# The start row of the routing counts as a 128-row bf16 multiply instead of a one-row fp32 one

## The chip, the cores and the metric

The kernel runs on one core of one Trainium2 chip. The metric is the device time in microseconds (us); a lower time is better. The kernel before took 638.41 us, the median of three runs (637.21 to 638.51).

## The reference

Three stages follow one another: an attention with a sliding window and four sink keys (2 x 8 heads, 768 positions, head size 64), a mixture of 8 experts with a capacity, and a dense two-layer block with a leaky activation. The change touches the second stage, where each of 1536 tokens goes to one expert, greedily by the size of its logit, and no expert takes more than 192:

```python
cap = N // E
logits = x @ w_gate
order = np.argsort(-logits.flatten())
for idx in order:
    tok, e = (int(idx) // E, int(idx) % E)
    if assigned[tok] >= 0 or counts[e] >= cap:
        continue
    assigned[tok] = e
    counts[e] += 1
for e in range(E):
    mask = assigned == e
    h = np.maximum(x[mask] @ w1[e], 0.0)
    out[mask] = h @ w2[e]
```

The third stage is `(g @ w_out)` with `h = x @ w_in` and `g = max(h, 0) + alpha * min(h, 0)`.

## The kernel before

The program is written engine by engine, and the order of each engine's instructions is the order in the code; semaphores join the engines. Nothing is moved by a planner.

The greedy loop is done in eight rounds, r = 0 to 7. After each round one more expert is full. A round needs, for each free token, how many free tokens with a larger logit want each expert. VectorE compares the tokens' keys, one block of 128 tokens (a column c of 12) after another, into the 0/1 matrix `beats` (with `ties` for equal keys), and TensorE multiplies these with `want`, a 0/1 matrix of 128 x 9 for each block, and adds the results up in one PSUM region, `COUNTS` (12 blocks of 9 numbers, 108 columns). `count(r, c)` holds the 13 small matmuls of a column (L1392, L1394). Round 0 does the same by pieces, in `count_first_round` (L1397).

Before the first column, one matmul opens the accumulation with a start row: each of the 128 output rows gets the same 108 numbers, for each expert the number taken so far plus 1 - 192, and -3072 in the ninth place of each block. It is L1400 in round 0 and L1389 in rounds 1 to 6 (round 7 counts nothing), so it runs seven times. Its weights are `ones_row`, one row of 128 fp32 ones, and its moving data is `start_row`, one row of 108 fp32 numbers. GpSimd writes both once, among the constants in `routing_consts` (L498 to L519), during the attention. VectorE rewrites the expert part of `start_row` at the end of each round in `fill_expert` (L1048), from the loads in PSUM. TensorE, VectorE and ScalarE wait for all 23 constants (`consts_ready`) after the attention.

Where the rounds lie: rounds 0 and 1 come after the attention, with little else for TensorE to do; matmuls on zeros (`keep_clock`, L1233) are put between. From there on the rounds are woven into the matmuls of the experts and of the dense block, which go in four groups j of two experts. Round 2 begins after the fourth product of expert 1 (`routing_beside_expert`, L1522), round 4 after the fourth product of expert 3, and round 6 after the fourth of expert 5; rounds 3 and 5 begin in the dense block of group 0 and of group 1, at step f = 8 (`routing_beside_ffn`, L1562). L1505 is the first matrix of an expert, L1514 its second, L1602 the dense block's up projection, L1617 its down projection. `ones`, a 128 x 128 tile of bf16 ones, is there already: it is the weight of the sums over tokens in `before_and_loads` (L1445).

Of the kernel before, what the change touches and what calls it, by code (L numbers as in the profile page):

```python
# [19 lines left out]
BF16 = mybir.dt.bfloat16  # L20
# [7 lines left out]
N, DM = B * S, H * D  # L28
E, FE, FF = 8, 1024, 2048
P = 128  # L30
CAP = N // E
QB = S // P
STEPS = B * QB
NT = N // P
# [24 lines left out]
def program(nc, q_t, k_t, k_sink, v_rows, v_sink_d, wg_d, w1_d, w2_d, w_in_d, w_out_d, alpha_d, out, n_sink, window):  # L59
# [9 lines left out]
    with ctx:  # L69
# [10 lines left out]
        tri_before = sb("tri_before", [P, P], BF16)  # L80
        tri_after = sb("tri_after", [P, P], BF16)
        ones = sb("ones", [P, P], BF16)
        ones_row = sb("ones_row", [1, P])
        logit = sb("logit", [P, NT, E])
        zeros = sb("zeros", [P, 512], BF16)
        alpha = sb("alpha", [P, FC])
# [2 lines left out]
        full = sb("full", [P, E])  # L89
        full_pen = sb("full_pen", [P, E])  # L90

        start_row = sb("start_row", [1, NT, E + 1])
        free = sb("free", [P, NT])
        cap_val = sb("cap_val", [P, NT])
        expert_no = sb("expert_no", [P, NT, E])
# [368 lines left out]
        def _(pool):  # L464
# [33 lines left out]
            def routing_consts():  # L498

                nc.gpsimd.memset(tri_before[:, :], 1.0).then_inc(consts_ready, 1)  # L500
                nc.gpsimd.memset(tri_after[:, :], -1.0).then_inc(consts_ready, 1)
                affine(tri_before[:, :], ALU.is_gt, 0.0, [[1, P]], 0, -1, consts_ready, 4 + 2 + 1)
                affine(tri_after[:, :], ALU.is_gt, 0.0, [[-1, P]], 0, 1, consts_ready, 5 + 2 + 1)
                nc.gpsimd.memset(ones[:, :], 1.0).then_inc(consts_ready, 1)
                nc.gpsimd.memset(ones_row[:, :], 1.0).then_inc(consts_ready, 1)
                nc.gpsimd.memset(one[:, :], 1.0).then_inc(consts_ready, 1)
                nc.gpsimd.tensor_copy(ident_half[:, :], ident[:, :]).then_inc(consts_ready, 1)
                nc.gpsimd.iota(slot_iota[:, :], [[1, CAP]], base=1, channel_multiplier=0,
                               allow_small_or_imprecise_dtypes=True).then_inc(consts_ready, 1)
                nc.gpsimd.iota(expert_no[:, :, :], [[0, NT], [-1, E]], base=E, channel_multiplier=0,  # L510
                               allow_small_or_imprecise_dtypes=True).then_inc(consts_ready, 1)
                nc.gpsimd.memset(full[:, :], 0.0).then_inc(consts_ready, 1)
                nc.gpsimd.memset(full_pen[:, :], 0.0).then_inc(consts_ready, 1)
                nc.gpsimd.memset(start_row[:, :, 0:E], 1.0 - CAP).then_inc(consts_ready, 1)
                nc.gpsimd.memset(start_row[:, :, E], -2.0 * N).then_inc(consts_ready, 1)
                nc.gpsimd.memset(free[:, :], 1.0).then_inc(consts_ready, 1)
                nc.gpsimd.memset(cap_val[:, :], BIG).then_inc(consts_ready, 1)
                nc.gpsimd.memset(assigned[:, :, :], 0.0).then_inc(consts_ready, 1)
                nc.gpsimd.iota(token_no[:, :], [[P, NT]], base=0, channel_multiplier=1,  # L519
                               allow_small_or_imprecise_dtypes=True).then_inc(consts_ready, 1)  # L520
# [303 lines left out]
        def _(dve):  # L824
# [202 lines left out]
            def fill_expert(r):  # L1027

                e = r % 2
                dve.wait_ge(loads_counted, r + 1)
                chain.after(nc.vector.scalar_tensor_tensor(out=full_new[:, e, :], in0=LOADS, scalar=float(CAP),
                                                           in1=full[:, :], op0=ALU.is_ge, op1=ALU.subtract))
                nc.vector.tensor_tensor(out=numbered[:, :], in0=full_new[:, e, :], in1=expert_no[:, 0, :], op=ALU.mult)
                nc.vector.tensor_tensor(out=full[:, :], in0=full[:, :], in1=full_new[:, e, :], op=ALU.add)
                chain.after(nc.vector.tensor_tensor(out=lack[:, :, :], in0=assigned[:, :, :],
                                                    in1=full_new[:, e, :].unsqueeze(1).to_broadcast([P, NT, E]), op=ALU.mult))
                nc.vector.tensor_reduce(out=off[:, 0:1], in_=numbered[:, :], axis=AX, op=ALU.add)
                nc.vector.tensor_scalar(out=full_pen[:, :], in0=LOADS, scalar1=float(CAP), scalar2=-BIG,  # L1040
                                        op0=ALU.is_ge, op1=ALU.mult)
                chain.after(nc.vector.scalar_tensor_tensor(out=lack[:, :, :], in0=SLOTS, scalar=1.0, in1=lack[:, :, :],
                                                           op0=ALU.add, op1=ALU.mult))
                if r >= 2:
                    dve.wait_ge(w2_loaded[e], 16 * (r // 2))
                nc.vector.tensor_scalar(out=expert_of[e][:, :], in0=off[:, 0:1], scalar1=-1.0, scalar2=float(E),
                                        op0=ALU.mult, op1=ALU.add).then_inc(expert_known, 1)
                nc.vector.tensor_scalar(out=start_row[:, :, 0:E], in0=LOADS[0:1, :].unsqueeze(1).to_broadcast([1, NT, E]),  # L1048
                                        scalar1=1.0 - CAP, scalar2=None, op0=ALU.add).then_inc(room_ready, 1)
                chain.after(nc.vector.tensor_reduce(out=slot[:, :], in_=lack[:, :, :], axis=AX, op=ALU.add))  # L1050

# [176 lines left out]
        def _(pe):  # L1228
# [155 lines left out]
            def count(r, c):  # L1384
                if c == 0:
                    pe.wait_ge(want_ready, r + 1)
                    pe.wait_ge(room_ready, r)
                    pe.wait_ge(tok_ready, TURNS * r)
                    nc.tensor.matmul(COUNTS, ones_row[:, :], start_row[:, :, :], start=True, stop=False, skip_group_check=True)  # L1389
                pe.wait_ge(beats_ready, NT * (r - 1) + c + 1)  # L1390
                for t in range(NT):
                    nc.tensor.matmul(COUNTS[:, t, :], beats[:, c % 3, t * P:(t + 1) * P], want[:, c, :],  # L1392
                                     start=False, stop=False, skip_group_check=True)
                nc.tensor.matmul(COUNTS[:, c, :], ties[:, c % 3, :], want[:, c, :], start=False,  # L1394
                                 stop=(c == NT - 1), skip_group_check=True).then_inc(counted, 1)

            def count_first_round():  # L1397

                pe.wait_ge(want_ready, 1)
                nc.tensor.matmul(COUNTS, ones_row[:, :], start_row[:, :, :], start=True, stop=False, skip_group_check=True)  # L1400

                def count_low(g):

                    c, third = PIECES[LOWER[g]]
                    pe.wait_ge(low_ready, g + 1)
                    for i in range(4):
                        last = nc.tensor.matmul(COUNTS[:, c, :], low[:, g % LOWS, i * P:(i + 1) * P], want[:, 4 * third + i, :],
                                                start=False, stop=False, skip_group_check=True)
                    last.then_inc(low_counted, 1)

                lows = 0
                for n, (c, third) in enumerate(PIECES):
                    pe.wait_ge(pieces_ready, n + 1)
                    if c // 4 != third:
                        if lows >= 3:
                            count_low(lows - 3)
                        for i in range(4):
                            last = nc.tensor.matmul(LOW_BANK[lows % 3][:, i * P:(i + 1) * P], piece(n)[:, i * P:(i + 1) * P],
                                                    ident_half[:, :], start=True, stop=True)
                        last.then_inc(low_turned, 1)  # L1420
                        lows += 1
                    else:
                        nc.tensor.matmul(COUNTS[:, c, :], ties[:, c % 3, :], want[:, c, :], start=False, stop=False,
                                         skip_group_check=True)
                        if n < len(PIECES) - 4 and n >= 4:
                            keep_clock(1, spare)
                    for i in range(4):
                        last = nc.tensor.matmul(COUNTS[:, 4 * third + i, :], piece(n)[:, i * P:(i + 1) * P], want[:, c, :],
                                                start=False, stop=(n == len(PIECES) - 1 and i == 3), skip_group_check=True)
                    last.then_inc(pieces_read, 1) if n < len(PIECES) - 1 else last.then_inc(counted, NT)  # L1430
                    if n == len(PIECES) - 4:
                        for g in range(lows - 3, lows):
                            count_low(g)
# [274 lines left out]
```

## Time and profile before

| | |
|---|---|
| median of three runs | 638.41 us |
| the profiled execution's own time | 638.79 us |
| its span (first to last instruction) | 637.0 us |
| instructions | 12935 |
| TensorE matmuls busy | 620.3 us, 97% |
| VectorE busy | 419.9 us, 66% |
| ScalarE busy | 308.3 us, 48% |
| GpSimd busy | 196.5 us, 31% |
| mean granted clock of TensorE | 0.99 |

The busy time of the matmuls counts the time from the start to the end of each, and they overlap, so it isn't a time at full pace. The time that a matmul takes from the others is the distance of its start from the next one's. In a timeline, `PE` are matmuls and `PEld` weight loads; an fp32 matmul of the program stands there as two loads and two matmuls (x2). The bracket at the end of a row gives the idle time of the engine ahead of it and what ended it.

### The profile page before, as it was taken

How to read it: one execution, taken by the hardware profiler on the slowest of the kernel's cores; microseconds unless marked ns; L12 is line 12 of the kernel's file. 1: busy time of each engine (PE TensorE's matmuls, PEld its weight loads, DVE VectorE, ACT ScalarE, POOL GpSimd, SP SyncE). 2: the span in 40 equal slices, each digit the busy share in tenths (PEclk: the TensorE clock that was granted, in tenths of full speed). 3: DMA queues.
4: the chain of work that ended last, by engine and by line, in shares of the span. 5: the costliest groups of instructions: out<-in, count | busy, mean ns of one | idle time of the engine just before them, and what ended most of it. 6: DMA issues, size and time to landing. Idle time of an engine off the chain costs nothing.

```text
span 637.0 us, 12935 instructions
## 1 busy us (share of the span) xinstructions
PE 620.3 (97%) x4949; PEld 557.9 (88%) x4954; DVE 419.9 (66%) x1156; ACT 308.3 (48%) x716; POOL 196.5 (31%) x211
## 2 busy tenths in 40 slices
PE   8899999899999999999999999999999999999996
PEld 4789998759899888899999888999989989999995
DVE  7788887978576979844759798438587520035552
ACT  5888884511132655532236554322465642346663
POOL 4998881010111342111113431211233410113331
PEclk9899999889999999999999999999999999999999
DMA  7477854535450143037002510370016610000001
GB/s 260 150 256 274 273 192 157 191 94 198 139 203 1 67 158 116 2 104 253 35 2 85 206 51 2 117 273 1 2 67 227 243 75 17 1 1 1 1 1 50
DMA packets 31221, 72.37 MB, mean 114 GB/s; under 512 B 2876, under 2 KB 2936, under 8 KB 31160
## 3 DMA queue, kind: packets, MB, share of 16 engines
q1 hardware_dynamic: 27232, 60.69, 27.2%
q0 software_dynamic: 1984, 6.29, 2.9%
q10 hardware_dynamic: 1944, 4.56, 2.0%
q8 instruction: 40, 0.66, 0.4%
q14 instruction: 21, 0.17, 0.1%
HBM read 65.22 MB, written 6.32 MB: 112 GB/s over the span
## 4 chain that ended last, share of the span: by engine, by line
PE 76%; DVE 3%; DMA 1%; issue 0%; POOLq 0%; POOL 0%; ACT 0%
PE bank L1602 21%; PE bank L1617 21%; PE bank L1514 14%; PE bank L1505 13%; PE bank L1392 3%; DVE beats L971 1%; DMA rank_row<-key_row 1%; PE bank L1483 1%; PE bank L1461 1%; DVE beats L942 1%; PE bank L1233 1%; PE bank L1445 0%; PE bank L1438 0%; PE bank L1394 0%; DVE ties L984 0%
## 5 line engine op out<-in xcount | busy, mean ns | idle before, releaser
L603 POOL TENSOR_TENSOR wi_lo<-w_in,wi_hi 128x512 fp32r<-128x512 f32 x64 | 89.2, 1396 | 274.4 <-ACT wi_hi L744 274.4
L942 DVE TENSOR_SCALAR beats<-rank_row,key 128x512 bf16<-128x512 f32 (+11 forms) x144 | 92.3, 661 | 12.4 <-PE bank L1394 12.4
L1617 PE MATMUL bank<-wo_lo,g_hi 128*128 128x512 f32 x192 | 76.0, 396 | 0.0
L1617 PE MATMUL bank<-wo_hi,g_lo 128*128 128x512 f32 x192 | 75.7, 394 | 0.0
L1617 PE MATMUL bank<-wo_hi,g_hi 128*128 128x512 f32 x192 | 75.5, 393 | 0.0
L1215 DVE SCALAR_TENSOR_TENSOR g<-bank,g_neg 128x384 f32<-128x384 f32 x64 | 35.5, 554 | 52.9 <-ACT g_neg L796 52.9
L794 ACT ACTIVATE g_neg<-bank 128x384 f32<-128x384 f32 x64 | 31.4, 491 | 79.9 <-PE bank L1602 79.1
L1602 PE MATMUL bank<-y_hi,wi_hi 128*128 128x384 f32 x256 | 57.8, 347 | 0.0
L770 ACT ACTIVATE h_t<-bank 128x192 f32<-128x192 f32 x64 | 21.1, 330 | 74.2 <-PE bank L1505 71.3
L670 ACT ACTIVATE prob<-neg_s,neg_max 128x260 f32<-128x260 f32 x96 | 48.9, 510 | 15.4 <-DVE neg_max L853 13.2
L1602 PE MATMUL bank<-y_lo,wi_hi 128*128 128x384 f32 x256 | 55.2, 336 | 0.0
L1602 PE MATMUL bank<-y_hi,wi_lo 128*128 128x384 f32 x256 | 54.8, 334 | 0.0
L1205 DVE TENSOR_TENSOR g_lo<-g,g_hi 128x384 fp32r<-128x384 f32 x64 | 44.5, 695 | 14.7 <-ACT g_hi L801 14.5
L1083 DVE TENSOR_TENSOR y_lo<-bank,y_hi 128x192 fp32r<-128x192 f32 x32 | 11.3, 354 | 60.3 <-ACT y_hi L781 59.8
L781 ACT CAST y_hi<-bank 128x192 fp32r<-128x192 f32 x32 | 10.2, 318 | 77.5 <-PE bank L1514 77.5
L1514 PE MATMUL bank<-h_t,w_b 128*128 128x192 f32 x256 | 47.7, 334 | 0.0
L1602 PEld LDWEIGHTS bank<-y_hi,wi_hi 128*128 128x128 f32 x256 | 44.1, 188 | 3.4 <-ACT y_hi L781 0.2
L1602 PEld LDWEIGHTS bank<-y_lo,wi_hi 128*128 128x128 f32 x256 | 46.2, 188 | 0.0
L1505 PE MATMUL bank<-x_gt,w_b 128*128 128x192 f32 x256 | 45.3, 330 | 0.7 <-ACT x_gt L760 0.7
L1199 DVE TENSOR_TENSOR wo_lo<-w_out,wo_hi 128x512 fp32r<-128x512 f32 x64 | 45.8, 715 | 0.0
L1602 PEld LDWEIGHTS bank<-y_hi,wi_lo 128*128 128x128 f32 x256 | 45.4, 188 | 0.0
L801 ACT CAST g_hi<-g 128x384 fp32r<-128x384 f32 x64 | 32.8, 513 | 24.9 <-DVE g L1215 20.3
(180 smaller groups left out, 1369.3 us busy)
## 6 DMA issues: line engine op xcount, KB each, us to landing
w_a<-moe_w SPq DMA_DIRECT2D x8, 1024.0 KB, 5.2
w_a<-moe_w SPq DMA_DIRECT2D x4, 2048.0 KB, 11.3
w_b<-moe_w SPq DMA_DIRECT2D x8, 1024.0 KB, 5.2
w_b<-moe_w SPq DMA_DIRECT2D x4, 2048.0 KB, 10.2
k_raw<-k_t SPq DMA_DIRECT2D x11, 512.0 KB, 4.8
q_raw<-q_t SPq DMA_DIRECT2D x11, 512.0 KB, 3.9
w_in<-moe_w_in SPq DMA_DIRECT2D x8, 512.0 KB, 5.0
w_out<-moe_w_out SPq DMA_DIRECT2D x8, 512.0 KB, 4.7
```

The lines of the kernel that those rows point to most:

```text
L603: nc.gpsimd.tensor_tensor(out=wi_lo[:, f % 2, :, :], in0=w_in[:, :, f * P:(f + 1) * P], in1=wi_hi[:, f % 2, :, :].bitcast(F32), op=ALU.sub ...
L670: nc.scalar.activation(prob[b][:, h, :], neg_s[:, h % 4, :], ACT.Exp, bias=neg_max[b][:, h:h + 1], scale=-1.0, accum_out=p_sum[b][:, h, 0: ...
L794: nc.scalar.activation(g_neg[:, :], UP_BANK[f % 2][:, 0:GS], ACT.Relu, scale=-1.0).then_inc(neg_turned, 1)
L801: nc.scalar.copy(g_hi[:, f % 3, :], g[:, f % 2, :]).then_inc(g_hi_done, 1)
L942: return nc.vector.tensor_scalar(out=beats[:, c % 3, lo:hi], in0=rank_row[:, lo:hi], scalar1=key[:, c:c + 1], scalar2=None, op0=op)
L1199: nc.vector.tensor_tensor(out=wo_lo[:, f % 2, :], in0=w_out[:, f, :], in1=wo_hi[:, f % 2, :].bitcast(F32), op=ALU.subtract).then_inc(wo_sp ...
L1205: nc.vector.tensor_tensor(out=g_lo[:, f % 3, :], in0=g[:, f % 2, :], in1=g_hi[:, f % 3, :].bitcast(F32), op=ALU.subtract).then_inc(g_split, 1)
L1215: nc.vector.scalar_tensor_tensor(out=g[:, f % 2, :], in0=u, scalar=0.0, in1=g_neg[:, :], op0=ALU.max, op1=ALU.add).then_inc(g_ready, 1)
L1505: last = nc.tensor.matmul(into, w1[e][:, c, k * P:(k + 1) * P], x_gt[e][:, c, :], start=(c == 0), stop=(c == DC - 1))
L1514: last = nc.tensor.matmul(into, w2[e][:, f, m * P:(m + 1) * P], h_t[e][:, f, :], start=(f == 0), stop=(f == EC - 1))
L1602: last = nc.tensor.matmul(UP_BANK[f % 2][:, 0:GS], w[:, f % 2, c, :], y[:, c, :], start=(n == 0), stop=(n == len(passes) - 1))
L1617: last = nc.tensor.matmul(DOWN_BANK[t][:, :], a[:, f % 3, t * P:(t + 1) * P], w[:, f % 2, :], start=(f == 0 and n == 0), stop=(f == FC - 1 ...
```

## The change

The start row's tile becomes 128 rows of bf16, all zero but the first, which holds the same numbers as before. It is multiplied with the 128 x 128 tile of ones in place of the single fp32 row of ones. The tile of fp32 ones is dropped. GpSimd zeroes the whole new tile first, waits for that, and then writes the first row. VectorE writes the first row as bf16. The numbers (-191 to 1, and -3072) can all be written in bf16.

```diff
-        ones_row = sb("ones_row", [1, P])
-        start_row = sb("start_row", [1, NT, E + 1])
+        start_row = sb("start_row", [P, NT, E + 1], BF16)
 ...
-                nc.gpsimd.memset(ones_row[:, :], 1.0).then_inc(consts_ready, 1)
 ...
-                nc.gpsimd.memset(start_row[:, :, 0:E], 1.0 - CAP).then_inc(consts_ready, 1)
-                nc.gpsimd.memset(start_row[:, :, E], -2.0 * N).then_inc(consts_ready, 1)
+                nc.gpsimd.memset(start_row[:, :, :], 0.0).then_inc(consts_ready, 1)
+                pool.wait_ge(consts_ready, 17)
+                nc.gpsimd.memset(start_row[0:1, :, 0:E], 1.0 - CAP).then_inc(consts_ready, 1)
+                nc.gpsimd.memset(start_row[0:1, :, E], -2.0 * N).then_inc(consts_ready, 1)
 ...
-                nc.vector.tensor_scalar(out=start_row[:, :, 0:E], in0=LOADS[0:1, :].unsqueeze(1).to_broadcast([1, NT, E]),
+                nc.vector.tensor_scalar(out=start_row[0:1, :, 0:E], in0=LOADS[0:1, :].unsqueeze(1).to_broadcast([1, NT, E]),
 ...
-                    nc.tensor.matmul(COUNTS, ones_row[:, :], start_row[:, :, :], start=True, stop=False, skip_group_check=True)
+                    nc.tensor.matmul(COUNTS, ones[:, :], start_row[:, :, :], start=True, stop=False, skip_group_check=True)
 ...
-                nc.tensor.matmul(COUNTS, ones_row[:, :], start_row[:, :, :], start=True, stop=False, skip_group_check=True)
+                nc.tensor.matmul(COUNTS, ones[:, :], start_row[:, :, :], start=True, stop=False, skip_group_check=True)
```

## Rows read from the trace of the kernel before

**Rows 1.** The page: the chain that ended last, shares of the span by engine.
```profile
PE 76%; DVE 3%; DMA 1%; issue 0%; POOLq 0%; POOL 0%; ACT 0%
```
**Rows 2.** Waits of the matmuls, 100 to 180.4 us: total, times, longest us.
```profile
PE bank L1423 <- DVE beats L971: 1.0, 2, 0.5
...
PE bank L1392 <- DVE beats L942: 0.3, 1, 0.3
```
**Rows 3.** Instructions on start_row: min/median/max ns, first and last start in us.
```profile
L1389 PEld LDWEIGHTS bank<-start_row,ones_row x12: 181/182/184, 142.6 to 429.7; 1*128 1x128 f32 x12
L1389 PE MATMUL bank<-start_row,ones_row x12: 270/312/355, 142.6 to 429.7; 1*128 1x108 f32 x12
L1048 DVE TENSOR_SCALAR start_row<-bank x8: 234/235/235, 133.1 to 483.9; 1x96 f32<-1x96 f32 x8
L1400 PEld LDWEIGHTS bank<-start_row,ones_row x2: 181/182/184, 115.8 to 115.9; 1*128 1x128 f32 x2
```
**Rows 4.** Timeline of the matmuls, round 4, ahead of columns 0 and 1.
```profile
304.51 0.33 PE L1505 MATMUL bank<-x_gt,w_b 128*128 128x192 f32 x1
304.77 0.47 PE L1389 MATMUL bank<-start_row,ones_row 1*128 1x108 f32 x2
305.17 0.28 PE L1392 MATMUL bank<-want,beats 128*128 128x9 bf16 x5
...
306.73 0.33 PE L1505 MATMUL bank<-x_gt,w_b 128*128 128x192 f32 x1
306.89 0.45 PE L1392 MATMUL bank<-want,beats 128*128 128x9 bf16 x12
```
**Rows 5.** Timeline of the matmuls, round 3, ahead of columns 0 and 1.
```profile
235.99 0.40 PE L1617 MATMUL bank<-wo_lo,g_hi 128*128 128x512 f32 x1
236.32 0.47 PE L1389 MATMUL bank<-start_row,ones_row 1*128 1x108 f32 x2
236.72 0.23 PE L1392 MATMUL bank<-want,beats 128*128 128x9 bf16 x3
...
241.11 0.40 PE L1617 MATMUL bank<-wo_lo,g_hi 128*128 128x512 f32 x1
241.35 0.46 PE L1392 MATMUL bank<-want,beats 128*128 128x9 bf16 x12
```
**Rows 6.** Timeline around a sum with the tile of bf16 ones.
```profile
279.91 0.33 PE L1505 MATMUL bank<-x_gt,w_a 128*128 128x192 f32 x1
280.07 0.50 PE L1445 MATMUL bank<-assigned,ones 128*128 128x96 bf16 x12
280.43 0.20 PE L1448 MATMUL bank<-assigned,tri_before 128*128 128x96 bf16 x1
280.47 0.39 PE L1505 MATMUL bank<-x_gt,w_a 128*128 128x192 f32 x1
```
**Rows 7.** Timeline, starts of rounds 0, 1 and 2.
```profile
116.64 0.10 PEld L1423 LDWEIGHTS bank<-want,ties 128*128 128x128 bf16 x1 [0.17 <-DVE beats L971]
...
143.35 0.31 PE L1392 MATMUL bank<-want,beats 128*128 128x9 bf16 x6 [0.28 <-DVE beats L942]
...
180.39 0.19 PEld L1392 LDWEIGHTS bank<-want,beats 128*128 128x128 bf16 x5 [0.29 <-DVE beats L942]
```
**Rows 8.** Timeline of GpSimd, the constants.
```profile
97.37 0.17 POOL L518 MEMSET assigned<- 128x96 bf16 x1
...
102.16 0.50 POOL L531 COPY sink_p<-prob 128x32 f32<-128x32 f32 x3 [4.54 <-ACT prob L670]
```
**Rows 9.** Windows: PE busy, granted clock, DMA share, GB/s.
```profile
126.50:129.90 3.40, 2.31 (x29) 1.00 0.02 5
129.90:133.30 3.40, 3.25 (x21) 0.50 0.00 0
...
140.20:143.60 3.40, 3.12 (x25) 1.00 0.24 47
```
**Rows 10.** The page, groups of instructions: one of the long matmuls' groups, busy us, mean ns.
```profile
L1602 PE MATMUL bank<-y_hi,wi_hi 128*128 128x384 f32 x256 | 57.8, 347 | 0.0
```

## The prediction

> **What bounds the kernel now.** I read the page's chain of waits first, then what TensorE waited for by stretch, then the timelines around each start row. The chain that ended last lies on TensorE for 76% of the span, with VectorE at 3% and DMA at 1% far behind [rows 1]. The waits say where this is not so. Between 100 and 180.4 us the matmuls wait on VectorE's comparisons in rounds 0 and 1 [rows 2], and on ScalarE's copies for some tenths more; the same query from 180.4 us to 636 us has no row at all. So after 180.4 us every tenth of a microsecond taken out of TensorE's stream should come off the end, and before it only what is not followed by a wait. What matters of a matmul there is the distance between its start and the next start, not its duration.
>
> **What the change removes.** Seven start rows in fp32: one at L1400 (round 0) and six at L1389, each shown as two loads of 181 to 184 ns and two matmuls [rows 3]. In round 4 the last expert matmul ahead of it starts at 304.51 and the first count matmul behind it at 305.17, 0.66 us. One column later the same two instructions, with no start row between, are at 306.73 and 306.89, 0.16 us. The start row costs 0.50 us there [rows 4]. In round 3 it is 235.99 to 236.72, 0.73 us, against 241.11 to 241.35, 0.24 us: 0.49 us [rows 5]. Rounds 5 and 6 repeat rounds 3 and 4 (at 361.1 and 429.5 us, with the same distances to 0.01 us). Of the 0.50 us, 0.40 are the two passes and 0.10 lie ahead of the first (304.51 to 304.77 is 0.26, not 0.16).
>
> **What it adds on TensorE.** One bf16 matmul of 108 columns with 128 x 128 weights. The nearest row is the sum with the same tile of ones: L1448, 96 columns in bf16, starts at 280.43 and the next matmul at 280.47, 0.04 us, and the first of the twelve L1445 follows the expert's matmul by 0.16 us, as a count does [rows 6]. Both also write into the bank of the counts. Scaled to 108 columns, 0.04 x 108 / 96 = 0.045 us. The low end is the mean of the twelve L1445, of 96 down to 8 columns: 0.36 / 12 = 0.03 us. The high end is that the bf16 matmul keeps the 0.10 us ahead of it and pays 0.10 us more where the counts begin, as if the passage and not the shape cost them: 0.245 us. I take 0.045, since L1445 and L1448 show neither.
>
> So a start row on the path saves 0.50 - 0.045 = 0.455 us beside an expert and 0.49 - 0.045 = 0.445 us beside the dense block.
>
> **Which of the seven are on the path.** Round 0: right behind the start row TensorE catches up with VectorE and waits 0.17 us at 116.64 [rows 7]. It reaches that wait earlier by 0.45 us and leaves it at the same time. Gain 0, as VectorE's comparisons hide it. Round 1: the first count waits until 143.35 for the comparison, 0.28 us after the start row has ended [rows 7]. Gain 0. Round 2: the first count waits for its comparison at 180.39 [rows 7], on which VectorE had started once the keys' row had come by DMA. Gain 0. Rounds 3 to 6 have no such wait. The sum is 2 x 0.445 + 2 x 0.455 = 1.80 us. If the cover of rounds 0 to 2 were gone, each would bring another 0.45.
>
> **What is late next.** After 236 us VectorE, ScalarE and GpSimd are released by TensorE's own results, so they come earlier with it. Arriving 0.45 us sooner asks more of what was computed ahead. In round 4 VectorE had the first three comparisons ready long before: it is idle until the first column has been counted. I see no wait of any size on TensorE in this part, so I count nothing back; if the first comparison of each of the four rounds were late by the whole gain, all 1.80 us would go.
>
> **The other parts.** VectorE's write of the row (235 ns, eight times, [rows 3]) keeps its 96 elements and its source in PSUM; bf16 instead of fp32 out changes little. I bound it at 0.05 us either way; it is on VectorE's path in rounds 0 and 1 only, so 0 to 0.1 us in sum, taken as 0. GpSimd drops the memset of one row of 128 and adds one of 128 x 108 in bf16, like the 0.17 us of `assigned` (128 x 96), with a wait for it in front of the next. That is at most 0.3 us more (the memset, and as much again for the wait) on an engine that then idles for 4.54 us [rows 8]; the attention's GpSimd work behind it waits for ScalarE anyway. Consumers read the constants after 111 us, 14 us later. Cost 0. If the cover were gone it would be 0.3 us. No instruction passes a DMA, and no DMA is touched. No engine waits longer for anything in the new code but GpSimd for itself.
>
> The tiles allocated behind the two shrunken ones move down by 512 + 216 bytes in each partition. No row shows that an address matters, and none excludes it; see the rivals.
>
> **A rule that speaks against the size.** Two fp32 loads of one row take 181 to 184 ns [rows 3], like the 188 ns of loads of 128 rows. The Trainium skill, "TensorE: Matmul & The Clock Gate", section "LDWEIGHTS (loading the stationary operand)", says that a load's time goes by its columns and that the number of rows does not matter. The duration agrees, and from this one would expect a one-row fp32 matmul to fit into the stream as any other. The starts do not agree: 0.20 us from pass to pass at 108 columns. By the rule alone I would expect a saving below 0.2 us a round, under 0.8 us in all. The sum above does not use the rule.
>
> **The sum.** The profiled execution took 638.79 us, its span is 637.0 us, and 1.8 us lie around it. The span would become 635.2 us and that execution 637.0 us. It stood 0.4 us above the median of the runs, 638.41 us, from which the change gives 638.41 - 1.80 = 636.6 us, 0.28% less.
>
> **The rivals.**
> The seam stays. The bf16 matmul costs 0.245 us (above), so a round saves 0.25 us and the four 1.0 us: 637.4 us, no change that can be told. For it: the 0.10 us ahead of the start row appears in each of the places. Against it: L1445 opens its accumulation with 128 rows and shows 0.16 us [rows 6].
>
> The gain is given back to a comparison or to a copy somewhere behind 236 us, in whole: 638.4 us. For it: VectorE is at 66%. Against it: no wait of the matmuls there.
>
> The clock. Between rounds 0 and 1 lies a stretch of 3.4 us with a granted clock of 0.50 (1.2 GHz), and it follows one in which the matmuls were busy for 2.31 of 3.40 us [rows 9]; round 0 has another such pair, with the 0.50 in 119.7:123.1. The change takes matmul time out of just that region, 0.45 us each at 115.8 and 142.6 us. If the stretch 140.20 to 143.60 (3.12 us busy, [rows 9]) loses the clock for the next one, expert 0's products, which fill TensorE, run at half rate for 3.4 us and lose 1.7 us: 636.6 + 1.7 = 638.3 us. Against it: 3.12 - 0.45 = 2.67 is still above the 2.31. The Trainium skill, "TensorE: Matmul & The Clock Gate", section "HAM oscillation — how this bites in real kernels", says that idle gaps of the array send it back to the slow clock; the order of the rows agrees, and whether the change crosses that point no row can show.
>
> Slower: the addresses. From 145 us to the end 2368 matmuls of the experts and the dense block follow each other with little between (three groups of 256 at L1602, of which one is [rows 10], three of 192 at L1617, and 1024 at L1505 and L1514). If the tiles' new places cost each of them more than (1.80 + 1.28) / 2368 = 1.3 ns, the kernel is slower by over 0.2%; at 2 ns it is +4.7 - 1.8 = +2.9 us, 641.3 us. Against it: the cost would have to fall on nearly all of these tiles at once. For it: only that nothing here excludes it, and it could as well be a gain.
>
> **How the numbers follow.** Chances: forecast 0.60; seam 0.08; given back 0.07; clock 0.11; addresses worse 0.08, better by 1 ns or more (634 us) 0.06. A measurement of this kernel can tell about 0.2%, 1.28 us, from no change. The forecast is only 0.5 us beyond that, so a tenth of it counts as no change. Faster: 0.54 + 0.06 = 0.60. No change: 0.06 + 0.08 + 0.07 + 0.08 (clock) = 0.29. Slower: 0.08 + 0.03 (clock lost twice) = 0.11. The forecast's own range is 636.0 to 637.4, from the bounds of the bf16 matmul and the spread of the runs. The range reaches to the clock's and the given back case: 635.7 to 638.7.
>
> **What would show it.** Right: one load and one matmul at L1389, `128*128 128x108 bf16`, with 0.16 us (round 4) and 0.24 us (round 3) ahead of it and 0.04 to 0.05 us behind it; waits on VectorE longer by 0.45 us in rounds 0 to 2; starts in the dense block of group 1 earlier by about 0.9 us and at the end by 1.8 us. Wrong: a wait at L1392 in rounds 3 to 6, 0.1 us or more between the start row and the first count, a third stretch at 0.50, or other starts than before between matmuls of L1505 or L1617.

## The result

The changed kernel takes 636.02 us (median of 12 runs, 635.22 to 637.14) against 638.35 us (12 runs, 637.21 to 639.25): a ratio of 0.9963, with a 95% interval of 0.9955 to 0.9971. That is 2.3 us less, by the interval 1.8 to 2.9 us. The forecast was 1.8 us less, 636.6 us, which is the low end of that interval.

The profiled execution took 635.48 us. Its page begins

```profile
span 633.6 us, 12921 instructions
...
PE 614.9 (97%) x4942; PEld 554.5 (88%) x4947; DVE 418.6 (66%) x1156; ACT 308.5 (49%) x716; POOL 196.5 (31%) x211
```

The span is 3.4 us shorter, more than the 2.3 us between the medians, so two single profiles don't tell the size; where the rest lies is told below. The instructions on `start_row` (duration min/median/max, first and last start) answer to [rows 3]: one load and one matmul a round, in bf16, and VectorE's write longer by 5 ns.

```profile
L1048 DVE TENSOR_SCALAR start_row<-bank x8: 240/240/242, 132.3 to 480.6; 1x96 bf16<-1x96 f32 x8
L1389 PEld LDWEIGHTS bank<-start_row,ones x6: 96/98/98, 141.2 to 426.4; 128*128 128x128 bf16 x6
L1389 PE MATMUL bank<-start_row,ones x6: 211/211/222, 141.4 to 426.5; 128*128 128x108 bf16 x6
```

The timeline of the matmuls (start, duration) at round 4, as in [rows 4]:

```profile
302.66 0.21 PE L1389 MATMUL bank<-start_row,ones 128*128 128x108 bf16 x1
302.71 0.45 PE L1392 MATMUL bank<-want,beats 128*128 128x9 bf16 x12
```

and at round 3, as in [rows 5]:

```profile
234.42 0.40 PE L1617 MATMUL bank<-wo_lo,g_hi 128*128 128x512 f32 x1
234.66 0.22 PE L1389 MATMUL bank<-start_row,ones 128*128 128x108 bf16 x1
234.72 0.45 PE L1392 MATMUL bank<-want,beats 128*128 128x9 bf16 x12
```

In round 3 the passage from the down projection to the counts takes 0.30 us where it took 0.73, and the start row is 0.24 us behind its predecessor, as the count of the next column is. In round 4 the start row holds TensorE for 0.05 us, and the passage takes 0.21 us (0.66 before). From the last long matmul ahead of round 3's start row to the first count of round 6, over all four start rows on the path, it is 234.42 to 426.59 us now, 192.17, and was 235.99 to 429.95, 193.96: 1.79 us less, where 1.80 was the sum. The four passages up to the first count give 1.75 of it (0.43 and 0.445 us, twice each). The rest lies one matmul further on: the second count starts 0.039 us behind the first in the kernel before, and 0.028 us in the changed one.

Before 180.4 us the matmuls wait more (total, times, longest), which answers to [rows 2]:

```profile
PE bank L1423 <- DVE beats L971: 1.5, 3, 0.5
...
PE bank L1392 <- DVE beats L942: 0.6, 1, 0.6
```

The saved time of rounds 0 and 1 has become wait on VectorE's comparisons there, as said: 0.5 us more in round 0, 0.35 us more in round 1 (0.63 us where it was 0.28). From 180.4 us on the same query is empty, as before. The constants on GpSimd:

```profile
96.37 0.10 POOL L511 MEMSET full_pen<- 128x8 f32 x1
96.40 0.18 POOL L512 MEMSET start_row<- 128x108 bf16 x1
96.64 0.17 POOL L514 MEMSET start_row<- 1x96 bf16 x1
...
101.56 0.51 POOL L531 COPY sink_p<-prob 128x32 f32<-128x32 f32 x3 [4.42 <-ACT prob L670]
```

The zeroing and its wait are 0.24 us (96.40 to 96.64), and GpSimd then idles for 4.42 us instead of 4.54 [rows 8]: 0.1 us, covered.

### The profile page after: what moved, and what is told of

Read it like the earlier page. It is cut to its first block, busy times and chain, and to the rows that moved or that the text cites. A ratio compares the mean times of both kernels' runs of the same rounds, so it can differ in the third digit from the quotient of the medians.

```text
span 633.6 us, 12921 instructions
## 1 busy us (share of the span) xinstructions
PE 614.9 (97%) x4942; PEld 554.5 (88%) x4947; DVE 418.6 (66%) x1156; ACT 308.5 (49%) x716; POOL 196.5 (31%) x211
## 4 chain that ended last, share of the span: by engine, by line
PE 78%; DVE 2%; issue 0%; ACT 0%; POOLq 0%; POOL 0%; DVEq 0%
PE bank L1602 22%; PE bank L1617 21%; PE bank L1514 14%; PE bank L1505 14%; PE bank L1392 3%; PE bank L1483 1%; PE bank L1461 1%; DVE beats L971 1%; DVE beats L942 0%; PE bank L1418 0%; PE bank L1445 0%; PE bank L1233 0%; PE bank L1438 0%; PE bank L1394 0%; DVE in_slot L1055 0%
## 5 line engine op out<-in xcount | busy, mean ns | idle before, releaser
L781 ACT CAST y_hi<-bank 128x192 fp32r<-128x192 f32 x32 | 10.2, 319 | 77.5 <-PE bank L1514 77.5
L1505 PE MATMUL bank<-x_gt,w_b 128*128 128x192 f32 x256 | 45.3, 330 | 0.7 <-ACT x_gt L760 0.7
## 6 DMA issues: line engine op xcount, KB each, us to landing
w_a<-moe_w SPq DMA_DIRECT2D x4, 2048.0 KB, 10.3
w_b<-moe_w SPq DMA_DIRECT2D x4, 2048.0 KB, 10.2
```

The source lines that it names most:

```text
L1505: last = nc.tensor.matmul(into, w1[e][:, c, k * P:(k + 1) * P], x_gt[e][:, c, :], start=(c == 0), stop=(c == DC - 1))
```

## The experiments

All times are compared with runs of the kernel before on the same chip. The last column comes from the traces: how far an instruction of VectorE behind the first count of round 6 has moved towards the start, less the same for one shortly before round 3, both against the first profile of before. It holds what rounds 3 to 6 bring and nothing from ahead of them.

| kernel | median us | before us | ratio, 95% interval | rounds 3 to 6 in the trace, us |
|---|---|---|---|---|
| the changed kernel, first | 636.02 | 638.35 | 0.9963 (0.9955, 0.9971) | -1.80 |
| again | 636.12 | 639.11 | 0.9957 (0.9942, 0.9973) | -1.80 |
| late_only | 636.41 | 639.11 | 0.9963 (0.9950, 0.9975) | -1.75 |
| early_only | 638.22 | 639.11 | 0.9989 (0.9978, 1.0000) | +0.03 |
| padded | 636.18 | 639.11 | 0.9960 (0.9947, 0.9973) | -1.79 |
| one_row_bf16 | 637.27 | 638.12 | 0.9986 (0.9975, 0.9997) | -1.00 |
| rows128_fp32 | 636.68 | 638.12 | 0.9980 (0.9969, 0.9991) | -1.22 |
| fp32_twice | 639.22 | 638.12 | 1.0013 (1.0001, 1.0025) | +0.87 |
| bf16_nine | 637.89 | 638.12 | 0.9992 (0.9981, 1.0002) | -0.25 |
| fewer_zeros | 636.94 | 638.20 | 0.9975 (0.9965, 0.9986) | -1.79 |
| before_a, before_b (one run each) | 638.02, 637.35 | 638.20 | | 0.00, 0.00 |
| again_b (one run) | 636.30 | 638.20 | | -1.79 |

**again.** The changed kernel, unchanged.

> The changed kernel once more, beside the kernel before. Theory A (only the start rows of rounds 3 to 6 lie on the path, 0.45 us each): 1.8 us below the kernel before. Theory B (part of the gain comes from rounds 0 to 2, by the clock or by VectorE): 2.3 us below, as in the first measurement.

The interval (1.7 to 3.7 us less) holds both, so the times alone can't part A from B. In its trace rounds 3 to 6 bring 1.80 us once more.

**late_only and early_only.** Both kinds of start row are there; a round picks one.

```diff
+        def in_bf16(r):
+            return r >= 3        # early_only: r < 3
 ...
-                nc.vector.tensor_scalar(out=start_row[0:1, :, 0:E],
+                nc.vector.tensor_scalar(out=(start_row if in_bf16(r + 1) else start_one)[0:1, :, 0:E],
 ...
+                if in_bf16(r):
                     nc.tensor.matmul(COUNTS, ones[:, :], start_row[:, :, :], ...)
+                else:
+                    nc.tensor.matmul(COUNTS, ones_row[:, :], start_one[:, :, :], ...)
```

> bf16 start rows with 128 rows in rounds 3 to 6, fp32 with one row in rounds 0 to 2. Theory A: the whole gain of 1.8 us, as in the changed kernel; in the trace 0.16 us (rounds 4 and 6) and 0.24 us (3 and 5) ahead of the row and 0.05 behind. Theory B: 1.8 us, but 0.5 us less than the changed kernel in the same comparison.

> bf16 start rows in rounds 0 to 2, fp32 in rounds 3 to 6. Theory A: no difference from the kernel before (within 0.2 us), with longer waits of the first count on VectorE in rounds 1 and 2 (by 0.45 us). Theory B: 0.5 us below the kernel before.

late_only has nearly the whole gain, early_only a small one whose interval ends at zero (0 to 1.4 us). So the four late start rows are the bulk. But the longer wait of the first count in round 2, which theory A wants, is missing in early_only; the timeline of its matmuls:

```profile
179.34 0.21 PE L1394 MATMUL bank<-start_row,ones 128*128 128x108 bf16 x1
179.38 0.45 PE L1406 MATMUL bank<-want,beats 128*128 128x9 bf16 x12
```

No wait lies between them, so here round 2's start row was on the path, too.

**padded.** The tiles behind get their old addresses back.

```diff
         ones = sb("ones", [P, P], BF16)
+        pad_a = sb("pad_a", [P, P])
 ...
         start_row = sb("start_row", [P, NT, E + 1], BF16)
+        pad_b = sb("pad_b", [P, NT * (E + 1)], BF16)
```

> The changed kernel with two unused tiles of 512 and 216 bytes where the dropped bytes were, so that all other tiles have the addresses of the kernel before. Theory A: the same time as the changed kernel. Rival C (part of the change comes from the new addresses): 0.5 us or more away from it, and other distances between the matmuls of L1505 or L1617.

It is the changed kernel to 0.01 us in rounds 3 to 6, and its median is within 0.1 us of that of again, on the same chip. The rival of the addresses is out.

**one_row_bf16 and rows128_fp32.** The change has two halves, the type and the number of rows. Each kernel has one of them.

```diff
 one_row_bf16:
-        start_row = sb("start_row", [P, NT, E + 1], BF16)
+        start_row = sb("start_row", [1, NT, E + 1], BF16)
-                    nc.tensor.matmul(COUNTS, ones[:, :], start_row[:, :, :], ...)
+                    nc.tensor.matmul(COUNTS, ones[0:1, :], start_row[:, :, :], ...)
 rows128_fp32:
+        start_row = sb("start_row", [P, NT, E + 1])
+        ones_full = sb("ones_full", [P, P])
+                    nc.tensor.matmul(COUNTS, ones_full[:, :], start_row[:, :, :], ...)
```

> One row, but in bf16 (the first row of the tile of ones as weights). Theory R (the fp32 row is dear because a one-row matmul doesn't overlap with its neighbours: 0.10 us ahead, its load exposed, and 0.10 us behind): 0.2 us a start row, so about 0.25 us saved in each of rounds 3 to 6, 1.0 us in all. Theory D (it is dear because it is fp32): 0.05 us a start row, 1.8 us in all, like the changed kernel.

> 128 rows, but in fp32 (a 128 x 128 tile of fp32 ones, and a start row of 128 x 108 fp32). Theory R: two passes of 0.09 to 0.11 us and nothing around them, 0.2 us a start row, so 0.3 us saved in each of rounds 3 to 6, 1.2 us in all. Theory D: 0.5 us a start row as in the kernel before, no gain.

Theory R holds in both sizes. At round 4, first the one row in bf16 and then the 128 rows in fp32, in the timelines of their matmuls (the last start of the product ahead of them is at 302.89 and at 303.13 us):

```profile
303.15 0.22 PE L1387 MATMUL bank<-start_row,ones 1*128 1x108 bf16 x1
303.30 0.31 PE L1390 MATMUL bank<-want,beats 128*128 128x9 bf16 x6
```

```profile
303.30 0.37 PE L1391 MATMUL bank<-start_row,ones_full 128*128 128x108 f32 x2
303.50 0.24 PE L1394 MATMUL bank<-want,beats 128*128 128x9 bf16 x4
```

One row in bf16: 0.26 us ahead and 0.15 behind, 0.41 in all. 128 rows in fp32: 0.16 ahead and 0.20 for the two passes, 0.37 in all. The kernel before has 0.66, the changed one 0.21. So of the 0.45 us the type alone brings 0.25 and the rows alone 0.29, and each brings less where the other is done already (0.16 and 0.20). In bf16 the shape costs TensorE 0.10 us on entering the one-row matmul and 0.10 us on leaving it, and the 0.01 us at the second count comes with it: it is there with one row of bf16 (0.038 us) and gone with 128 rows of fp32 (0.028 us).

**fp32_twice.** The fp32 start row of the kernel before, issued twice in rounds 1 to 6 (`for _ in range(2):` around L1389).

> The kernel before with the fp32 one-row start row issued twice in rounds 1 to 6 (the second overwrites the first). The second one costs its two passes of 0.20 us. Theory A (rounds 3 to 6 on the path, 1 and 2 covered for 0.28 and 0.19 us): 4 x 0.40 + 0.12 + 0.21 = 1.9 us above the kernel before. If all rounds were covered: 0. If none were: 2.4 us.

A miss: 0.9 us in rounds 3 to 6, not 1.6, and 1.1 us more in the medians, not 1.9. Timeline at round 4:

```profile
304.93 0.69 PE L1390 MATMUL bank<-start_row,ones_row 1*128 1x108 f32 x4
```

The starts of its four passes are 0.197, 0.112 and 0.111 us apart, and the count follows after 0.202. The second row costs 0.22 us, not 0.40: its two passes are 0.11 us each between passes of their own shape. The 0.20 us of [rows 4] from pass to pass are 0.11 us and about 0.09 for the change of shape: once in the first pass, beside the 0.10 ahead of it, and once at the exit.

**bf16_nine.** The bf16 start row nine times in rounds 1 to 6.

> The changed kernel with the bf16 start row issued nine times in rounds 1 to 6. Eight more of 0.045 to 0.048 us each are 0.36 to 0.38 us a round; rounds 1 and 2 have 0.6 us of cover, so 4 x 0.37 = 1.5 us above the changed kernel, 0.3 us below the kernel before (with 1.8 us for the change). If a bf16 start row cost 0.1 us: 3.2 us above the changed kernel.

A hit: 1.55 us above the changed kernel in rounds 3 to 6 (1.80 - 0.25), with starts 0.047 and 0.048 us apart. Its median is 0.2 us below the kernel before, with an interval (1.2 less to 0.1 more) that holds no change. Nine of the new rows cost about as much as one old one.

**before_a, before_b and again_b.** Further traces of the two kernels.

> The kernel before, unchanged, once more, for the trace. Theory E: the first count of round 2 waits for a DMA whose arrival differs from run to run, so that the fp32 start row of round 2 is on the path in some runs: 0.66 us from the last product's start to the first count if the DMA is early, up to 1.0 us if it is late. Theory A as predicted: always a wait there (over 0.66 us). In both the distances of rounds 3 to 6 stay 0.73, 0.66, 0.73 and 0.66 us.

> The kernel before a second time: as for the first. The stretches of slow clock (1.2 GHz) before 145 us lie elsewhere or are missing if they go by the run; if the fp32 start rows set them, they are where the first profile has them.

> The changed kernel a third time, for the trace: 0.21 us at the bf16 start rows of rounds 4 and 6 and 0.30 at 3 and 5, whatever the clock does before 145 us; in round 2 between 0.21 us (DMA early, theory E) and 1.0 us.

The distances of rounds 3 to 6 are those foreseen in all three. In round 2 both copies of before waited (1.12 and 0.82 us in all), and so did the first profile (0.84). again_b needed 0.43, again 0.60 and the first profile of the changed kernel 0.38. The slow stretches go by the run: before_a and before_b have one of 6.8 us, from 118.4 and 118.0 us, and none at 130 us, unlike the first profile [rows 9].

**fewer_zeros.** The clock, put to use: in the chain of waits of the first profile of before, the 14 matmuls on zeros ahead of the first choice of tokens are on the path for 3.81 us, as the slow stretch of [rows 9] falls on them:

```profile
131.88 3.81 PE bank L1233 x14
```

```diff
-            keep_clock(14, spare)
+            keep_clock(9, spare)
```

> The changed kernel with 9 instead of 14 matmuls on zeros ahead of the first choice of tokens. Theory F (a slow stretch that falls on these 14 makes them the path, by 0.5 us, as at 131.88 to 135.68 us in the trace of before): their 5 are 1.1 us at the fast clock and 2.1 us at the slow one, so the choice waits for VectorE whatever the clock, and the kernel is 0.3 to 0.5 us below the changed one on average. Rival: the missing matmuls bring a further slow stretch and cost 0.5 to 1.7 us.

Theory F missed, and the time is in the rival's range: 636.94 us, some 0.8 us above the changed kernel by the ratios, though the intervals (0.9965 to 0.9986 and 0.9955 to 0.9971) overlap. Its timeline:

```profile
133.99 1.19 PE L1461 MATMUL bank<-token_no,in_slot 128*128 128x1 f16 x24 [1.33 <-DVE in_slot L1055]
135.34 1.06 PE L1233 MATMUL bank<-zeros 128*128 128x512 bf16 x3 [0.16 <-issue]
136.19 4.33 PE L1374 MATMUL bank<-ident,key 128*128 128x128 f32 x24
```

TensorE now idles for 1.33 us, a slow stretch follows at 135.8 us, and the 24 passes that spread the keys take 4.33 us, where they take 2.94 us in the first profile of before. VectorE waits for these, and from VectorE's write of `key` in round 1 to the turned keys of round 2 it is 32.59 us here and 31.67 or 31.68 us in the 13 other traces: the stretch cost 0.92 us. Whether the missing zeros brought such a stretch in most runs, one trace can't show, but the mean granted clock leans that way: 0.987 to 0.992 in the eleven executions (mean 0.989), against 0.987 to 0.996 in the first twelve of the changed kernel (mean 0.991); the six of again have a mean of 0.9925. A single stretch of 3.4 us at half clock is 0.0027 of such a mean. The zeros also had little to give back. From VectorE's update of `assigned` to its reading of the chosen tokens it is 5.86 us in the first profile of before, but 5.34 to 5.38 us in ten of the 13 traces with 14 zeros, and 5.34 us with 9 zeros. The 0.5 us that theory F wanted to save are in one trace of 13.

## Why the prediction was right

**The sum.** Rounds 3 to 6 were forecast at 0.445 and 0.455 us, 1.80 in all, and every trace of the changed kernel has 1.79 or 1.80. The parts are nearly as read: 0.16 and 0.24 us ahead, 0.047 us behind at round 4 (0.045 foreseen), no new wait. In round 3 the distance behind is 0.058 us, 0.013 us over the forecast; the second count's 0.011 us, which no term foresaw, makes up for it. That the sum agrees to 0.01 us has this bit of luck in it.

**Rounds 0 and 1** bring nothing, by late_only and by the longer waits. The first count of round 1 starts 1.06 us after the last matmul on zeros in the first profile of before and in late_only, and as well in the changed kernel. Up to the keys of round 2 no gain can be seen either: they are turned at 169.0, 168.0 and 167.6 us in the three traces of before and at 167.9, 168.4 and 168.8 us in the three of the changed kernel.

**Round 2: the step that was too simple.** "Gain 0" rested on one trace. The count waits for a comparison, the comparison for the keys' row, and that comes by a DMA whose arrival differs by 1.4 us between the 14 traces (8.9 to 10.3 us after the keys were turned). Where it is early, the start row is on the path, as in early_only. The comparison started 10.0 to 10.3 us behind in the three traces of before and 9.6 to 9.8 us in the three of the changed kernel. In all six a wait was left, so each passage is as long as the arrival makes it: in these six and in late_only, padded and fewer_zeros it is the start of the comparison less 9.19 us. But the passage can't be shorter than 0.66 us with the old start row (rounds 4 and 6), and it is 0.38, 0.60 and 0.43 us in the changed kernel. The first of them, in the timeline of the changed kernel:

```profile
178.42 0.10 PEld L1389 LDWEIGHTS bank<-start_row,ones 128*128 128x128 bf16 x1
178.58 0.21 PE L1389 MATMUL bank<-start_row,ones 128*128 128x108 bf16 x1
...
178.79 0.46 PE L1392 MATMUL bank<-want,beats 128*128 128x9 bf16 x12
```

With the old row each of the three would have been 0.66 us, so the new one brought 0.06 to 0.28 us there, 0.19 us on average. The averages differ by 0.46 us (0.93 to 0.47): these 0.19 are the row, the other 0.27 are the arrival. Put as a rule of this passage: the old row is on the path where the comparison starts less than about 9.85 us behind the keys, which it does in 9 of the 14 traces, and it costs its whole 0.45 us below 9.40 us, as in early_only (9.1 us).

So "gain 0" was wrong for round 2 in the runs of the changed kernel, and right only for arrivals as late as those of before. Row and arrival together are as much as the measured 2.3 us have over the 1.8, as far as three traces of each kernel show it; the share of the arrival is luck unless the change has a part in it. What is left can't be told from the region before 140 us, where the copies of one program differ by up to 1.4 us.

What the arrival goes with can be seen. On SP's queue the second half of the next expert's first weights waits for the gathered tokens; it was issued 2.51 to 2.74 us after the keys were turned, and the row's load by ScalarE always after 2.92. Over the 14 traces the weights' issue and the row's arrival go together (correlation -0.93): the later the megabyte of weights, the earlier the row. In before_a, then in early_only (DMA issues and the comparison that ends the wait):

```profile
170.50 0.37 SPq L449 DMA_DIRECT2D w_b<-moe_w  x1
170.91 0.41 ACTq L718 DMA_DIRECT2D rank_row<-key_row  x1
...
178.31 0.35 DVE L951 SCALAR_TENSOR_TENSOR ties<-rank_row,key,tri_after 128x128 bf16<-128x128 f32 x1 [6.70 <-DMA rank_row<-key_row]
```

```profile
171.33 0.37 SPq L453 DMA_DIRECT2D w_b<-moe_w  x1
171.56 0.36 ACTq L726 DMA_DIRECT2D rank_row<-key_row  x1
...
177.74 0.35 DVE L959 SCALAR_TENSOR_TENSOR ties<-rank_row,key,tri_after 128x128 bf16<-128x128 f32 x1 [5.47 <-DMA rank_row<-key_row]
```

The row takes 7.4 us from issue to comparison in the one and 6.2 in the other. Its DMA packets run for 2.9 us in both; what differs is when the first of them starts, 4.0 us after the issue in before_a and 2.8 us in early_only. That the weights' packets, which start 1.0 us after their issue in both, hold up the row's is the likely reason, but it is not shown: no run moved the weights' load on purpose. It also stays open whether the change itself has a part in when the row arrives: its three traces (9.6 to 9.8 us) and those of before (10.0 to 10.3) don't overlap, but late_only and fp32_twice, both with fp32 in rounds 0 to 2, have 10.2 and 9.2 us.

**The rule on loads.** The sum went by the distance of the starts against the Trainium skill's "TensorE: Matmul & The Clock Gate", section "LDWEIGHTS (loading the stationary operand)", by which the number of rows does not matter to a load. Of its duration that is so (181 to 184 ns for one row of fp32, 186 to 192 ns for the 128 rows of L1505). Of the stream it isn't: the two shapes differ by 0.20 us in bf16 and 0.29 us in fp32. By that rule alone the prediction expected a gain under 0.8 us, and the type alone is worth 0.58 us in rounds 3 to 6 where both kernels have 128 rows (1.80 less the 1.22 of rows128_fp32).

**The rivals.** The seam did not stay. Its 0.245 us is just what one_row_bf16 costs, so it belongs to the one-row shape. Nothing was given back behind 236 us. The addresses don't matter (padded). The clock did not turn against the change: between 100 and 145 us the traces of both kernels have 3.4 or 6.8 us of slow clock, in places that go by the run. The argument against this rival was weak all the same: 2.67 us of matmuls was held to be safe, being above 2.31, but in the first profile of before the clock of 0.50 from 119.7 us follows a stretch with 2.64 us busy, and in that of the changed kernel the one from 119.4 us follows 2.67 (windows of the matmuls):

```profile
116.00:119.40 3.40, 2.67 (x53) 1.00 1.04 400
119.40:122.80 3.40, 3.16 (x57) 0.50 0.20 72
```

The slow stretches do move a single profile: from the last comparisons of round 0 to the choice of tokens the first profiles of the two kernels differ by 0.52 us, and before_a and before_b from the first profile of before by just as much.

## What to carry to other kernels

Read the price of a small matmul from the distance of the starts around it, set against the same passage without it, and not from its duration. A matmul whose weights have one row, set among matmuls of 128 rows, pays on entry and on exit, so zero rows that make it like its neighbours are cheaper than none; and fp32 pays again by its two passes. Where a wait hides a saving, ask what the wait is for: if it ends on a DMA, look at more than one trace before the saving is put at nothing, and compare the shortest passage that the old instruction allows with those of the new one.

## What was not expected of the hardware

The change of shape between 128 rows and one row costs 0.10 us each way in bf16. In fp32 it costs 0.09 ahead of the first pass, 0.09 in it and 0.09 at the exit. By contrast a passage from fp32 to bf16 at 128 rows costs nothing that can be seen behind 192 columns (0.16 us from the product's last start to a bf16 matmul, its own pace), and 0.02 us behind 108 (0.11 us, where its own two passes are 0.09 us apart). A one-row fp32 pass of 108 columns takes 0.11 us behind another of its shape.
